# Attention with two dense stages behind it: ten of twelve chunks come in one transfer instead of two

## The reference, cut to what matters

```python
for b in range(nb):
    intra = einsum('bhic,bhjc->bhij', qb, kb) * Dmask        # scores, decayed
    intra = einsum('bhij,bhjd->bhid', intra, vb)
    inter = einsum('bhid,bhde->bhie', qb * lam_pow, kv_state)
    out[:, :, sl] = intra + inter
    kv_state = lam_block * kv_state + einsum('bhsd,bhse->bhde', kb * rev_pow, vb)
```

## Time and profile before

| | us |
|---|---|
| time, median of 3 runs | 280.61 (280.56 to 280.8) |
| the profiled execution's own time | 282.59 |
| its span, first to last instruction | 280.8 |
| TensorE busy in the span | 270.9 |
| VectorE busy | 167.2 |
| ScalarE busy | 126.8 |
| GpSimd busy | 35.1 |

### The profile page before, as it was taken

The page is one execution under the profiler, slowest core; times in us unless marked ns, Lnnn a source line. Parts: engine busy times, 40 slices in busy tenths (PEclk is TensorE's granted clock), DMA queues, the critical chain, the costliest instruction groups (busy, mean ns, idle before and its releaser), DMA issues.

```text
span 280.8 us, 4274 instructions
## 1 busy us (share of the span) xinstructions
PE 270.9 (96%) x1740; PEld 225.4 (80%) x1740; DVE 167.2 (60%) x253; ACT 126.8 (45%) x229; POOL 35.1 (12%) x30
## 2 busy tenths in 40 slices
PE   8689699999999999999999999999999999999996
PEld 7578587888888888888888888888888888888885
DVE  4839899875868012546696753526987599515000
ACT  2256755948686112437731134567325404522121
POOL 0763573006800000000000000000000000000000
PEclk9999999999999999999999999999999999999999
DMA  7999999100000000000000000170000000300213
GB/s 285 396 345 317 402 360 392 62 0 0 2 0 0 0 2 0 0 0 2 1 0 0 4 0 0 42 259 0 0 0 2 0 0 0 114 37 0 112 75 114
DMA packets 7506, 23.35 MB, mean 83 GB/s; under 512 B 960, under 2 KB 1216, under 8 KB 7488
## 3 DMA queue, kind: packets, MB, share of 16 engines
q1 hardware_dynamic: 7344, 23.07, 22.1%
q10 hardware_dynamic: 144, 0.02, 0.0%
HBM read 19.94 MB, written 3.15 MB: 82 GB/s over the span
## 4 chain that ended last, share of the span: by engine, by line
PE 92%; DMA 3%; issue 1%; POOL 1%; DVE 0%; ACT 0%
PE ps L689 27%; PE ps L687 27%; PE ps L688 27%; PE ps L755 3%; PE ps L703 3%; DMA qk<-in_qk 3%; PE ps L740 2%; PE ps L720 2%; DVE qdec L592 0%; POOL kdec L268 0%; POOL qd L280 0%; ACT out_sb L395 0%
## 5 line engine op out<-in xcount | busy, mean ns | idle before, releaser
L687 PE MATMUL ps<-xk_h,wk_h 128*128 128x512 f32 x96 | 37.5, 390 | 0.0
L688 PE MATMUL ps<-xk_l,wk_h 128*128 128x512 f32 x96 | 37.4, 389 | 0.0
L689 PE MATMUL ps<-xk_h,wk_l 128*128 128x512 f32 x96 | 37.3, 389 | 0.0
L687 PE MATMUL ps<-kk_h,wv_h 128*128 128x512 f32 x96 | 37.3, 389 | 0.0
L688 PE MATMUL ps<-kk_l,wv_h 128*128 128x512 f32 x96 | 37.3, 389 | 0.0
L689 PE MATMUL ps<-kk_h,wv_l 128*128 128x512 f32 x96 | 37.3, 389 | 0.0
L538 DVE SCALAR_TENSOR_TENSOR kk_f<-ps,ring 128x512 f32<-128x512 f32 x24 | 16.6, 692 | 29.3 <-ACT ring L348 29.3
L562 DVE SCALAR_TENSOR_TENSOR gate<-x,prm,gate 128x512 f32<-128x512 f32 x48 | 32.6, 747 | 0.0
L348 ACT ACTIVATE ring<-ps 128x512 f32<-128x512 f32 x24 | 14.4, 601 | 31.9 <-PE ps L689 31.7
L365 ACT ACTIVATE gate<-x,prm 128x512 f32<-128x512 f32 x12 | 8.7, 727 | 42.6 <-DVE x L548 42.6
L687 PEld LDWEIGHTS ps<-xk_h,wk_h 128*128 128x128 f32 x96 | 18.0, 188 | 3.9 <-issue 0.2
(11 more groups left out here) (71 smaller groups left out, 507.2 us busy)
## 6 DMA issues: line engine op xcount, KB each, us to landing
qk<-in_qk SPq DMA_DIRECT2D x12, 512.0 KB, 6.1
kv<-in_kv SPq DMA_DIRECT2D x12, 512.0 KB, 8.3
out<-out_sb SPq DMA_DIRECT2D x11, 256.0 KB, 2.0
wk_raw<-in_w_k SPq DMA_DIRECT2D x4, 512.0 KB, 7.5
wv_raw<-in_w_v SPq DMA_DIRECT2D x4, 512.0 KB, 11.4
wr_raw<-in_w_r SPq DMA_DIRECT2D x2, 512.0 KB, 7.8
w_raw<-in_w_val SPq DMA_DIRECT2D x2, 512.0 KB, 4.4
w_raw<-in_w_out SPq DMA_DIRECT2D x2, 512.0 KB, 6.8
```

The lines of the kernel that those rows point to most:

```text
L687: nc.tensor.matmul(to, left(0), right(0), start=(i == 0), stop=False)
L688: nc.tensor.matmul(to, left(0), right(1), start=False, stop=False)
L689: done = nc.tensor.matmul(to, left(1), right(0), start=False, stop=(i == last))
```

## The change

Each chunk's four pieces are laid side by side in one tensor, 8 KB per partition and chunk. Chunks 0 and 1 still come in two transfers of 512 KB, each of which now reads 4 KB per partition out of 8 KB. Chunks 2 to 11 each come in one transfer of 1 MB. It increments the semaphore of the qk half alone; who waits for the kv half of such a chunk waits for that one. The buffers, their places and their number stay. The order of issue has qk(0), qk(1), kv(0), kv(1) first; a whole chunk then stands about where its qk half stood, and the pieces of the weights keep their places between the chunks.

```diff
-        qk = [place(f"qk_{i}", [P, 2, DM], kk_at + i * 8 * KB) for i in range(IN_BUFS)]
-        kv = [place(f"kv_{i}", [P, 2, DM], kk_at + i * 8 * KB + 4 * KB) for i in range(IN_BUFS)]
+        chunk = [place(f"chunk_{i}", [P, 4, DM], kk_at + i * 8 * KB) for i in range(IN_BUFS)]
+        qk = [z[:, 0:2, :] for z in chunk]
+        kv = [z[:, 2:4, :] for z in chunk]
...
+        def kv_wait(eng, n):
+
+            if n < 2:
+                eng.wait_ge(kv_here[n], 16)
+            else:
+                eng.wait_ge(qk_here[n % IN_BUFS], 16 * (n // IN_BUFS + 1))
...
+            def load_chunk(n):
+                free(n)
+                sp.dma_start(chunk[n % IN_BUFS][:, :, :], chunk_in[n]).then_inc(qk_here[n % IN_BUFS], 16)
...
             load_qk(0)
             load_qk(1)
             load_kv(0)
-            load_qk(2)
             load_kv(1)
-            load_qk(3)
-            load_kv(2)
-            load_kv(3)
-            load_qk(4)
+            load_chunk(2)
+            load_chunk(3)
+            load_chunk(4)
             load_weight(wk_raw, w_k, 0, wk_here)
-            load_kv(4)
-            load_qk(5)
+            load_chunk(5)
             load_weight(wk_raw, w_k, 1, wk_here)
-            load_kv(5)
-            load_qk(6)
-            load_kv(6)
-            load_qk(7)
+            load_chunk(6)
+            load_chunk(7)
             load_weight(wk_raw, w_k, 2, wk_here)
-            load_kv(7)
-            load_qk(8)
-            load_kv(8)
-            load_qk(9)
+            load_chunk(8)
+            load_chunk(9)
             load_weight(wk_raw, w_k, 3, wk_here)
-            load_kv(9)
-            load_qk(10)
-            load_kv(10)
-            load_qk(11)
+            load_chunk(10)
+            load_chunk(11)
             load_weight(wr_raw, w_r, 0, wr_here)
-            load_kv(11)
             load_weight(wr_raw, w_r, 1, wr_here)
...
-                    pool.wait_ge(kv_here[i], 16 * (n // IN_BUFS + 1))
+                    kv_wait(pool, n)
...
-                pe.wait_ge(kv_here[i], 16 * (n // IN_BUFS + 1))
+                kv_wait(pe, n)
...
-        "qk": np.stack([features(q), features(k)], axis=2),
-        "kv": np.stack([tokens(k[:, order]), tokens(v)], axis=2),
+        "chunk": np.stack([features(q), features(k), tokens(k[:, order]), tokens(v)], axis=2),
```

More of the change, by code:

```diff
@@ L46, in out_half, with build @@
     return row ^ (a >= PAIRS // 2)
-def build(nc, prm_in, qk_in, kv_in, w_k, w_v, w_r, w_val, w_out, out):
+def build(nc, prm_in, chunk_in, w_k, w_v, w_r, w_val, w_out, out):
     with ExitStack() as ctx:
@@ L130, in build @@
         qk_here = [sem(f"qk_here{i}") for i in range(IN_BUFS)]
-        kv_here = [sem(f"kv_here{i}") for i in range(IN_BUFS)]
+        kv_here = [sem(f"kv_here{i}") for i in range(2)]
         wk_here = [sem(f"wk_here{i}") for i in range(4)]
@@ L199, in load_qk @@
                 free(n)
-                sp.dma_start(qk[n % IN_BUFS][:, :, :], qk_in[n]).then_inc(qk_here[n % IN_BUFS], 16)
+                sp.dma_start(qk[n % IN_BUFS], chunk_in[n, :, 0:2, :]).then_inc(qk_here[n % IN_BUFS], 16)
             def load_kv(n):
                 free(n)
-                sp.dma_start(kv[n % IN_BUFS][:, :, :], kv_in[n]).then_inc(kv_here[n % IN_BUFS], 16)
+                sp.dma_start(kv[n % IN_BUFS], chunk_in[n, :, 2:4, :]).then_inc(kv_here[n % IN_BUFS], 16)
+            def load_chunk(n):
+                free(n)
+                sp.dma_start(chunk[n % IN_BUFS][:, :, :], chunk_in[n]).then_inc(qk_here[n % IN_BUFS], 16)
             def load_weight(raw, src, i, done):
```

## The result

The changed kernel takes 284.78 us (median of 4 runs, 283.55 to 285.13) against 280.59 (280.55 to 280.8): the ratio is 1.0122, with a 95% interval of 1.0083 to 1.0161. Run again beside the experiments it was at 1.0114 (1.0084 to 1.0143). The median of that repeat is 284.42 against 281.55. So it is slower, by 3.4 and 3.2 us by the two ratios, by 4.2 and 2.9 us by the two pairs of medians, and not within 0.2% of before, as the forecast of 281.1 had it. The profiled execution took 285.13 us with a span of 283.3, 2.5 more than before.

What follows compares the result with a forecast made beforehand. Attention before 49.40 us, with TensorE and DMA both nearly full, was taken to be set by the late qk of chunk 8; 1.23 - 0.78 = +0.45 us on 280.61 gave 281.06, rounded to 281.1, range 279.2 to 282.3.

Steps and rivals of the forecast that it cites:

- rival 1: 8 KB packets take twice 4 KB, so every half megabyte ahead of scores is paid: +1.39 us, 282.0; chance 0.28.
- (a): Chunks 0 and 1: first halves lead as before, kv(1) comes one transfer sooner; no gain.
- (b): Chunk 2: whole at 10.68, scores slip 0.65 us, still ahead of the update at 12.19; no cost, cover 0.34 us.
- (c): Chunk 7: scores 1.56 us late, pushing readiness for chunk 8 to 32.8, inside the hole; no cost by itself.
- (d): Chunk 8, which sets the end: scores wait for the kv half too, until 34.65 instead of 33.42, 1.23 us later.
- the hole before chunk 8: TensorE's idle 2.15 us before the scores of chunk 8, taken as what the transfers cost the end.
- (e): Chunk transfers: 8 KB packets take 309 ns instead of 323, saving 0.78 us over seven chunks up to chunk 8.
- (f): Chunks 10 and 11: chunk 10 whole at 40.5, just in time, chunk 11 at 43.1 to 43.8; no wait.
- 2: Rival: slow packets count by the packet, so half as many bring half of them; about -1.9 us, 278.7; chance 0.18.
- 3: Rival: the hole is the profiled execution's only, so the half megabyte comes from spare time; 0.0, 280.6; chance 0.17.
- 4: Rival: code loads wait for larger packets, growing the 1.02 us hole at 18.69; about +0.6 us, 281.2; chance 0.05.
- chunks 4 or 5 begin to wait: Sign in the attention that the whole prediction is wrong; no size given.

Runs made afterwards that it cites:

- e1_pitch: The kernel before, with all its 512 KB chunk transfers reading 4 KB per partition out of rows of 8 KB; ratio 1.0107 to the kernel before.
- e4_head: The changed kernel with chunks 0 and 1 from a tensor in which each half is contiguous; ratio 1.0051 to the kernel before.
- e13_pitch12k: As e4_head, but the halves of chunks 0 and 1 lie in rows 12 KB apart; ratio 1.0061 to the kernel before.
- e14_pitch8k256: As e4_head, but the halves of chunks 0 and 1 lie in rows 8 KB and 256 bytes apart; ratio 1.0078 to the kernel before.
- e11_flat: e4_head with the weight pieces laid contiguously as in e5_weights; ratio 1.0017 to the kernel before.
- e5_weights: The kernel before with each 512 KB piece of every weight laid contiguously; ratio 0.9962 to the kernel before, median 280.49 against 281.55 us.
- e3_joint: As e2_order, with scores and decay of q of chunks 2 to 11 also waiting for the kv half; ratio 1.0091 to the kernel before.
- e2_order: The kernel before with the change's order of issue, still in halves of 512 KB with a semaphore each; ratio 1.0000 to the kernel before.
- e12_flat_prm: e11_flat with the parameters issued first on SP's queue; ratio 1.0062 to the kernel before.
- e10_best: e5_weights with the parameters issued first on SP's queue; ratio 0.9954 to the kernel before, median 280.54 against 281.64 us.
- e6_4k: As e4_head, but the 1 MB transfers come in packets of 4 KB from two contiguous halves per chunk; ratio 1.0062 to the kernel before.
- e8_again: The changed kernel repeated unaltered, beside the other experiments; ratio 1.0114 to the kernel before, median 284.42 against 281.55 us.
- e7_warm: The changed kernel with seven more warm-up matmuls, three before the scores of chunk 0 and four after them; ratio 1.0107 to the kernel before.

## Why the prediction was wrong

The time lies outside the range (279.2 to 282.3), and rival 1, the slowest case of the list, gave 282.0.

**(a), chunks 0 and 1: this step failed.** It read "qk(0), qk(1) and kv(0) lead as before". The issue times do, the transfers don't. qk(0) landed at 4.2 before, and its scores start at 5.73 now. I had looked at order and bytes, and taken the new source, 4 KB out of rows of 8 KB, for equal. e1_pitch against before, and e4_head against the changed kernel, show that it costs, and the second pair shows how much: 1.8 us of the loss of 3.2 in the repeated set. e13_pitch12k and e14_pitch8k256 narrow it to the step of exactly 8 KB. Nothing in the trace of before shows such a step for the chunks, but its weight pieces were read in part rows all along (w_r at 8 KB, w_k at 16 KB), and a bound for it should have stood in the range.

**(b), chunk 2:** with (a) gone, its cover of 0.34 us is gone too. Its scores start at 12.75 instead of the 10.68 forecast, and the update at 12.19, named as the sign that (b) is wrong, moves to 13.93. e4_head, with the start mended, has it at 10.59.

**(c) and (d), the half megabyte before each score: the sign was right, the path was not, and the size is open.** It was 1.23 us at chunk 8 plus 0.16 at chunk 10. The runs measure 1.4 us (e4_head against before), 1.5 (e11_flat against e5_weights), 2.5 (e3_joint against e2_order) and 3.0 (e12_flat_prm against e10_best), each give or take about 1. So the term was right or about half of what it should have been. I had counted the landing of one chunk with everything ahead of it in place. But a later score also releases a buffer later, so the transfer three chunks on is issued later: the chain after shows this loop at chunks 5, 8 and 11, with the DMA engines idle before an issue (0.67 and 0.75). Nor does every profile have the hole before chunk 8 on which the sum stands: in e2_order, which takes the time of before, the scores of chunk 8 run at 31.20 without a wait. In e4_head four scores wait, those of chunks 2, 5, 6 and 8, 0.60, 0.94, 0.34 and 1.68 us. That its 1.4 us agree with 1.23 + 0.16 is luck in part.

**(e), the packets of 8 KB: right in its size, wrong in what it brings.** 310 ns measured against 309. e4_head and e6_4k are level, so the 0.78 us set against (d) do not show, though the intervals would hide them. Taken out, the forecast would have been +1.23 to +1.39, inside the interval of e4_head, and still less than half of the 3.2 us of the whole change, for want of (a).

**(f), no wait behind chunk 8:** wrong. The scores of chunk 11 wait until 46.19 for a transfer issued at 38.98.

**The rivals.** 1 had the right sign, with 1.39 us of the 3.2; the rest is (a), which no rival has. 2 and 3 are false: the order's half megabyte was not spare. 4 wasn't tested by itself; the hole in the middle of a chunk's scores, 1.02 us before, is 0.26 us of the weight loads in the profile after and 0.94 us in that of e8_again, so there it did not grow. The sign of what to look for was in the prediction's last sentence, that chunks 4 or 5 begin to wait; they do (0.33 and 0.37 us before their scores).

The profiled execution of before, 282.59 us, is 2 us above the median of its runs, that of the changed kernel, 285.13, is not. So the difference of the two profiles (+2.5) understates the timed one (+3.4 and +3.2 by the ratios).

## What to carry to other kernels

A larger transfer saves what its packets save, here 3 to 4% of DMA time in a full stretch; it costs the time by which its first byte's user now waits for its last, again and again where the next issue hangs on that user. That more buffers would break this loop is likely from the chain, but no run tried it. When a tensor is laid anew, count every transfer that now reads a part of a row, also those that were not to be changed, and look at the pitch. Before merging transfers, see whether the stream already shows slow stretches, and what in it is read in parts of longer rows: laying the weight pieces contiguously gained 0.4% here, where no run of the merged transfers beat the kernel before.

## What the runs showed of the hardware

- Reads of 4 KB per partition at a step of exactly 8192 bytes ran at 218 to 224 GB/s from 2 to 6 us (the changed kernel, e1_pitch, e7_warm, e8_again), contiguous ones at 346 to 381 (before, e2 to e6, e11_flat; 308 and 328 in e12_flat_prm and e10_best, with the parameters ahead on the queue), those at 12 KB or at 8 KB and 256 bytes at 351 and 355. The Trainium skill, page "DMA: Bandwidth & Descriptors", section "Latency and other measured facts", has copies of 16 KiB rows at 207 GB/s with a pitch of 512 KiB and at 103 with 4 MiB, full again with 4 KiB of padding and not with 192 bytes. Here the effect is there at 8 KB, and 256 bytes are enough for the rate.
- A packet of 8 KB took 310 ns against 2 x 161.5 for 4 KB, in loads of full stretches from the same queue; by the medians of all packets it is 309 against 2 x 159.
- TensorE, idle for 0.90 us before 5.73 and 0.83 us before 7.73, was granted 0.57 of its clock from 8 to 12 us, about half, which is the 1.2 GHz level for most of it (0.50 from 9 to 11 us). In another execution of the same code it was idle for 1.17 us and kept 1.00. Executions with a lower mean clock were the longer ones by their medians: 284.99 against 284.17 us in e8_again, 285.85 against 283.91 in e7_warm, 283.29 against 282.26 in e12_flat_prm, 282.93 against 281.19 in the kernel before beside e8_again.
